# Attention levels 2+3 and 4+5 of a chunked linear attention as one TensorE pass each

## The reference, cut to what matters

```python
def _attn_ref(r, k, v, w, u):        # (2, 8, 768, 48) each, u (8, 48)
    ...
    for t in range(S):
        kt, vt, rt, wt = (k[:, :, t], v[:, :, t], r[:, :, t], w[:, :, t])
        cur = np.einsum('bhd,bhe->bhde', u[None] * kt, vt)
        y[:, :, t] = np.einsum('bhd,bhde->bhe', rt, state + cur)
        state = wt[:, :, :, None] * state + np.einsum('bhd,bhe->bhde', kt, vt)

def _moe_ref(x, w_in, w_out):        # (1536, 384) x (384, 2048) x (2048, 384)
    h = np.maximum(x @ w_in, 0.0)
    return (h * h) @ w_out

def _moe2_ref(x, w_gate, w1, w2, capacity):
    ...                              # argmax of 8 experts, at most 384 rows each
    h = np.maximum(np.einsum('ecd,edf->ecf', disp, w1), 0.0)
    y = np.einsum('ecf,efd->ecd', h, w2)
    ...                              # rows back to their places, times the gate's value
```

## Time and profile before

| | us |
|---|---|
| median of 3 runs | 453.12 (451.08 to 453.23) |
| the profiled execution, its own time | 450.08 |
| its span, first to last instruction | 448.1 |
| TensorE matmuls busy | 427.2 (95%) |
| VectorE busy | 303.9 (68%) |
| ScalarE busy | 257.7 (58%) |
| GpSimd busy | 57.0 (13%) |

### The profile page before, as it was taken

One profiled execution on the slowest core, in us unless ns is written; L12 is line 12 of the kernel. 1 busy time (PEld: TensorE's weight loads), 2 busy tenths in 40 slices (PEclk: granted clock), 3 DMA queues, 4 the chain that ended last, 5 costly groups with the idle time before them and its releaser, 6 DMA issues.

```text
span 448.1 us, 14525 instructions
## 1 busy us (share of the span) xinstructions
PE 427.2 (95%) x5882; PEld 405.4 (90%) x5882; DVE 303.9 (68%) x763; ACT 257.7 (58%) x527; POOL 57.0 (13%) x77
## 2 busy tenths in 40 slices
PE   2899999999999999999999999999999899999994
PEld 2778999999999999999999999989997789999994
DVE  4996966766777767777778637558538877687510
ACT  3366766546644664466546665573648875686421
POOL 6400000000000200010001000301030333421201
PEclk9999999999999999999999999999999999999998
DMA  6847976850400131010001094522885998520001
GB/s 217 287 145 241 354 260 237 312 222 3 170 29 1 39 132 66 1 39 2 3 3 38 4 327 169 194 72 77 302 262 169 346 336 292 168 63 2 30 2 45
DMA packets 35642, 63.39 MB, mean 141 GB/s; under 512 B 3980, under 2 KB 21950, under 8 KB 35568
## 3 DMA queue, kind: packets, MB, share of 16 engines
q1 hardware_dynamic: 33120, 57.87, 38.0%
q0 software_dynamic: 2304, 4.47, 2.7%
q10 hardware_dynamic: 144, 0.00, 0.0%
HBM read 50.77 MB, written 14.19 MB: 145 GB/s over the span
## 4 chain that ended last, share of the span: by engine, by line
PE 87%; DVE 3%; issue 3%; ACT 2%; DMA 1%; POOL 1%; POOLq 0%; SPq 0%; DVEq 0%; ACTq 0%
PE bank L721 22%; PE bank L707 22%; PE bank L934 6%; PE pair L628 6%; PE bank L887 5%; PE pair L592 3%; PE pair L887 3%; PE pair L902 3%; PE bank L941 3%; PE bank L902 3%; PE pair L647 2%; PE pair L682 1%; DMA stage<-in_moe_w_in 1%; ACT W L973 1%; PE pair L934 1%
## 5 line engine op out<-in xcount | busy, mean ns | idle before, releaser
L707 PE MATMUL bank<-XH,W 128*128 128x256 f32 x576 | 118.7, 284 | 0.7 <-ACT RB L1077 0.7
L721 PE MATMUL bank<-W,GH 128*128 128x384 f32 x372 | 98.3, 345 | 0.0
L707 PEld LDWEIGHTS bank<-XH,W 128*128 128x128 f32 x576 | 94.9, 188 | 1.7 <-issue 0.9
L707 PE MATMUL bank<-XL,W 128*128 128x256 f32 x288 | 80.6, 280 | 0.0
L1280 DVE TENSOR_TENSOR GL<-GG,GH 128x256 fp32r<-128x256 f32 x96 | 40.4, 421 | 35.0 <-ACT GH L973 31.9
L1077 ACT ACTIVATE RB<-bank 128x256 f32<-128x256 f32 x96 | 36.6, 381 | 47.1 <-PE bank L707 46.0
L721 PEld LDWEIGHTS bank<-W,GH 128*128 128x128 f32 x372 | 61.7, 188 | 1.2
L721 PE MATMUL bank<-W,GL 128*128 128x384 f32 x186 | 62.6, 336 | 0.0
L973 ACT ACTIVATE GH<-GG 128x256 fp32r<-128x256 f32 x96 | 40.2, 418 | 34.1 <-PE bank L721 32.3
L707 PEld LDWEIGHTS bank<-XL,W 128*128 128x128 f32 x288 | 54.3, 189 | 0.0
L1217 DVE TENSOR_TENSOR KS<-KS 128x512 f32<-128x512 f32 x72 | 49.8, 693 | 6.1 <-PE pair L628 5.8
(11 more groups left out here) (164 smaller groups left out, 711.5 us busy)
## 6 DMA issues: line engine op xcount, KB each, us to landing
raw<-in_moe_w SPq DMA_DIRECT2D x23, 768.0 KB, 7.6
stage<-in_moe_w SPq DMA_DIRECT2D x9, 768.0 KB, 7.8
KS<-in_krw SPq DMA_DIRECT2D x12, 512.0 KB, 5.9
slots<-X SPq DMA_DIRECT2D x8, 579.0 KB, 6.5
VV<-in_v SPq DMA_DIRECT2D x12, 288.0 KB, 6.2
KS<-in_krw SPq DMA_DIRECT2D x12, 256.0 KB, 6.1
stage<-in_moe_w_in SPq DMA_DIRECT2D x4, 768.0 KB, 6.6
stage<-in_moe_w_out SPq DMA_DIRECT2D x4, 768.0 KB, 6.7
```

Source lines behind the costliest of these rows:

```text
L707: last = nc.tensor.matmul(bank[4 + f % 2][:, 0:2 * P], win[wa][:, c, f * P:(f + 1) * P], xa[:, c, :], start=n == 0, stop=n == 3 * KM - 1)
L721: last = nc.tensor.matmul(bank[6 + m][:, 0:DM], ga[(NF * g + f) % G3][:, cols], wout[wa][:, f, :], start=f == 0 and n == 0, stop=f == NF - ...
```

## The change

For groups 1 to 5, `two_levels(i, t, l)` takes the place of two levels, for l = 1 and l = 3 (PAIRS). A block of 4L tokens has quarters 0 to 3. The keys, decayed as for level l, meet three read quarters in one matmul of 96 moving columns per head and chunk: quarters 1 to 3 as they are (48 columns) and a second set from MIX[t] (48 columns), in which GpSimd has decayed the reads ahead (`reads_ahead`, two multiplies: quarters 2 and 3 into two places, then quarter 3 once more). VectorE's `select_pair` takes from the result with three predicated copies that wait for one another (3, 2 and 1 quarters, 384, 256 and 128 elements), with new masks mask4. The updates and totals stay as they were, one for each level. `two_levels` stands in slots 2 and 6 (levels were due in 1, 3, 5, 7); the updates of levels 2 and 4 in slots 3 and 7. Group 0 keeps its levels. GpSimd's program gets `group_ahead(n)`: groups 1 and 2 at the start of iteration 1, group g + 3 ahead of group g's scatters; the wait for the zeroed buffers moves to the first scatter. PAGE_PAD, semaphore steps on TensorE's queue in iteration 6, goes from 160 to 176. `pr` now shares the memory of `sc`.

```diff
-    PAGE_PAD = 160
+    PAGE_PAD = 176
...
-    LATER = (-1, 1, 3, 5, 7, 9, 10, 11, 12, 13)
+    LATER = (-1, 2, 3, 6, 7, 9, 10, 11, 12, 13)
+    PAIRS = (1, 3)
...
-            step(nc.gpsimd.tensor_tensor(mask[:, :, :], mask2[:, :, 0:C // 2], mask2[:, :, C // 2:C], ALU.add))
+            step(nc.gpsimd.tensor_tensor(mask[:, :, :], mask2[:, 1:, 0:C // 2], mask2[:, 1:, C // 2:C], ALU.add))
+            step(nc.gpsimd.tensor_tensor(low, mask2[:, 0, 0:C // 2], mask2[:, 0, C // 2:C], ALU.add))
...
+            def reads_ahead(n, t, l):
+
+                L, w = 1 << l, PAIRS.index(l)
+                done = 4 * (n - 1) + 2 * w
+                got = MIX[t].rearrange("p (g b j) -> p g b j", b=4, j=L)
+                x = KRW[t][n % 2][:, 0:XW].rearrange("p (g b j) -> p g b j", b=4, j=L)
+                td = totals(n, t, l).rearrange("p (g b o) -> p g b o", b=4, o=1)
+                pool.wait_ge(att[t], NSTEP * n + l)
+                pool.wait_ge(upd[t], NL * n + l)
+                pool.wait_ge(tot[t], NL * n + l)
+                nc.gpsimd.tensor_tensor(got[:, :, 1:3, :], x[:, :, 2:4, :],
+                                        td[:, :, 1:3, :].to_broadcast([P, XW // (4 * L), 2, L]),
+                                        ALU.mult).then_inc(ahead[t], 1)
+                pool.wait_ge(ahead[t], done + 1)
+                nc.gpsimd.tensor_tensor(got[:, :, 3, :], got[:, :, 2, :],
+                                        td[:, :, 1, :].to_broadcast([P, XW // (4 * L), L]),
+                                        ALU.mult).then_inc(ahead[t], 1)
...
             def body(i, attn, mlp, gate):
+                if i == 1:
+                    for n in (1, 2):
+                        group_ahead(n)
                 if gate:
                     g = i - 2
+                    if g + 3 < NG:
+                        group_ahead(g + 3)
...
+            def two_levels(i, t, l):
+
+                L = 1 << l
+                pe.wait_ge(ahead[t], 4 * (i - 1) + 2 * PAIRS.index(l) + 2)
+                pe.wait_ge(sel[t], NMASK * i + l)
+                x = KRW[t][i % 2]
+                apart = (2 - i % 2) * WIDTH - XW
+                n = C if (i, l) == (1, PAIRS[0]) else C - L
+                for q in range(HP):
+                    for h in range(2):
+                        for a in range(2):
+                            rows, c = slice(DP * a, DP * a + D), q * P + h * C
+                            to = half(h, a).start
+                            first = x[rows, c + L:c + L + 1]
+                            reads = bass.AP(first.tensor, first.offset,
+                                            [first.ap[0], [apart, 2], [4 * L, C // (4 * L)], [1, 3 * L]])
+                            last = nc.tensor.matmul(pair[t][to:to + n, a, q * P:q * P + 3 * C // 2],
+                                                    x[rows, XW + c:XW + c + n], reads, start=q == 0, stop=q == HP - 1)
+                last.then_inc(att[t], 2)
...
-                    elif k < NL:
+                    elif k < NL and (n == 0 or k == NL - 1):
                         level(n, t, k)
+                    elif k in PAIRS:
+                        two_levels(n, t, k)
...
+            def select_pair(i, t, l):
...
+                dve.wait_ge(att[t], NSTEP * i + l + 2)
+                dve.wait_ge(sel[t], NMASK * i + l)
+                if i == 1:
+                    dve.wait_ge(masked, 1)
+                take(1, 4, 0, 0).then_inc(part_sel[t], 1)
+                dve.wait_ge(part_sel[t], done + 1)
+                take(2, 4, 1, 0).then_inc(part_sel[t], 1)
+                dve.wait_ge(part_sel[t], done + 2)
+                take(3, 4, 1, 2).then_inc(sel[t], 2)
...
-                    if k < NMASK:
+                    if n > 0 and k in PAIRS:
+                        select_pair(n, t, k)
+                    elif n == 0 and k < NMASK:
                         select(n, t, k)
```

More of the change, by code:

```diff
@@ L116, in rwkv_moe_kernel @@
         mask2 = IN[0][0][:, :, :].rearrange("p h n -> p (h n)")[:, 0:NMASK * C].rearrange("p (l n) -> p l n", l=NMASK)
-        mask = sb("mask", [P, NMASK, C // 2], on=p1)
+        mask = sb("mask", [P, NMASK - 1, C // 2], on=p1)
+        mask4 = sb("mask4", [P, 2, 3 * C // 4], on=p1)
         eye = sb("eye", [P, C], on=p1)
@@ L206, in unsplit @@
             return x.rearrange("p (a b) -> p a b", a=parts)
-        made = sem("made")
+        made, masked = sem("made"), sem("masked")
         cleared = sem("cleared")
@@ L222, in rwkv_moe_kernel @@
         tot = [sem(f"tot{n}") for n in range(2)]
+        ahead = [sem(f"ahead{n}") for n in range(2)]
+        part_sel = [sem(f"part_sel{n}") for n in range(2)]
         sel = [sem(f"sel{n}") for n in range(2)]
@@ L512, in _ @@
             step(nc.gpsimd.tensor_tensor(eye[:, :], ident[:, 0:C], ident[:, C:P], ALU.add))
[L513 removed]
+            step(nc.gpsimd.tensor_tensor(mask[:, :, :], mask2[:, 1:, 0:C // 2], mask2[:, 1:, C // 2:C], ALU.add))
+            step(nc.gpsimd.tensor_tensor(low, mask2[:, 0, 0:C // 2], mask2[:, 0, C // 2:C], ALU.add))
             pool.wait_ge(cst, n_cst[0])
             odd = right_half(eye[:, :], 0)[:, :, 0]
[L516 removed]
+            nc.gpsimd.tensor_tensor(odd, odd, low, ALU.add).then_inc(made, 1)
             def first_totals(t, l):
@@ L531, in _ @@
                     first_totals(t, l)
+            step(nc.gpsimd.memset(wide4[:, :, :], 1.0))
+            pool.wait_ge(cst, n_cst[0])
+            for n, l in enumerate(PAIRS):
+                L = 1 << l
+                m = wide4[:, n, :].rearrange("p (g b j) -> p g b j", b=3, j=L)
+                step(nc.gpsimd.affine_select(out=m, in_=m, compare_op=ALU.is_ge, fill=0.0, base=0,
+                                             pattern=[[-4 * L, C // (2 * L)], [-L, 3], [0, L]], channel_multiplier=1))
+            pool.wait_ge(cst, n_cst[0])
+            for n, l in enumerate(PAIRS):
+                L = 1 << l
+                m = wide4[:, n, :].rearrange("p (g b j) -> p g b j", b=3, j=L)
+                step(nc.gpsimd.affine_select(out=m, in_=m, compare_op=ALU.is_ge, fill=0.0, base=L - 1,
+                                             pattern=[[4 * L, C // (2 * L)], [L, 3], [0, L]], channel_multiplier=-1))
+            pool.wait_ge(cst, n_cst[0])
+            nc.gpsimd.tensor_tensor(mask4[:, :, :], wide4[:, :, 0:3 * C // 4], wide4[:, :, 3 * C // 4:3 * C // 2],
+                                    ALU.add).then_inc(masked, 1)
             step(nc.gpsimd.memset(earlier[:, 0, :], 0.0))
@@ L1245, in select, with take @@
                     got.rearrange("p x (g j) -> p x g j", j=L)).then_inc(sel[t], 1)
+            def select_pair(i, t, l):
+                L, w = 1 << l, PAIRS.index(l)
+                done = 4 * (i - 1) + 2 * w
+                got = pair[t][:, :, :].rearrange("p a (q c) -> p (a q) c", q=HP)
+                to = AD[t][:, :, :].rearrange("p x (g b j) -> p x g (b j)", b=4, j=L)
+                m = mask4[:, w, :].bitcast(U32).rearrange("p (x g j) -> p x g j", x=1, j=3 * L)
+                def take(first, last, v, k):
+                    n = (last - first) * L
+                    return nc.vector.copy_predicated(
+                        to[:, :, :, first * L:last * L], m[:, :, :, 0:n].to_broadcast([P, H, C // (4 * L), n]),
+                        got[:, :, 3 * C // 4 * v:3 * C // 4 * (v + 1)].rearrange(
+                            "p x (g j) -> p x g j", j=3 * L)[:, :, :, k * L:k * L + n])
+                dve.wait_ge(att[t], NSTEP * i + l + 2)
[7 more added lines that the diff above has]
+                take(3, 4, 1, 2).then_inc(sel[t], 2)
             def heads(x):
```

14 lines of the change are left out of this document (11 added, 3 removed).

## The result

The changed kernel takes **464.06 us** (median; 461.92 to 466.57, 4 runs) against 453.11 us for the kernel before: a ratio of 1.0264, with a 95% interval from 1.0227 to 1.0302. It is 2.6% slower. The prediction said 451.8 us, with a range of 448.0 to 455.0, and gave 0.11 to "slower".

A forecast was written before the change was run, and what follows sets the result against it. TensorE, 95% busy, was taken as the bound, unless VectorE came late. Against the profiled 450.08 us: + 0.2 + 1.2 - 1.5 - 3 x 0.4 = -1.3, so 448.8, on the median's footing 451.8 us; range 448.0 to 455.0.

The forecast's parts named there:

- Until kk_rows (slot 10) may read the second tile: Iterations 3 to 5: VectorE's gapless queue up to kk_rows takes 11.8 us, against TensorE's 10.7.
- A: Moment at which the first tile's pass for levels 4+5 (slot 6) is done; both engines' times count from it.
- The wait at kk_rows: Iterations 3 to 5: TensorE waits about 1.1 us for VectorE before the transposes of kk_rows; none in iteration 2.
- the -0.4 for each of iterations 3 to 5: Net gain per iteration: 1.52 us saved on TensorE less a wait of 1.1 at kk_rows.
- the saving: TensorE per group: two wide passes take 3.06 us where four levels took 4.58, so 1.52 less; all kept in iteration 2.
- GpSimd against VectorE: GpSimd's multiplies slow a VectorE update by at most 0.04 us, mostly in slack; taken as 0.
- lock: Rival, 9%: shared-port lock makes VectorE's queue in iteration 1 2 us later; +2.0, total 453.8 us.
- Iteration 1: VectorE's queue delays level 5 and project(6), which follows at 58.05 instead of 56.85: +1.2 us, give or take 0.5.
- The pass: TensorE's wide pass of 64 records with 96 moving columns: 21 ns a record (16.1 to 25.8), 1.34 us plus 0.19.
- The trio: VectorE's three new dependent selects: 1.25 us against 0.68 for two old ones, 0.1 more for levels 2+3.
- The prologue: Preamble: one more small GpSimd add ahead of `made`, on which the first select waits: +0.2 us (0.1 to 0.3).
- 96 columns bind TensorE: Rival, 8%: two quadrants at once make 37 ns a record, a pass 2.4 us plus 0.19; total 459 us.

The follow-up runs named there:

- e1: Changed kernel with choice, ranks and place of groups 0 to 2 moved from slots 7, 8, 9 to 12, 13, 14: 455.22 us, ratio 1.0074.
- e5: Changed kernel with the late place of e1, and GpSimd's scatter of groups 0 and 1 held until the next group's first passes are through: 453.32 us.
- e2: Changed kernel with 12 unread products put ahead of the first tile's level 5 in iterations 3 to 5: 463.48 us.
- e8: The kernel of e2 with TensorE's empty instructions of iteration 6 cut from 176 to 101: 458.56 us, ratio 1.0154.
- e4: Changed kernel without GpSimd's multiplies ahead of the passes (decays on 48 of 96 read columns left out): 462.07 us, ratio 1.0225.
- e7: Kernel before with only late choice, ranks and place, and the scatter of groups 0 and 1 behind the next first passes: 454.60 us, ratio 1.0040.

## Why the prediction was wrong, step by step

**The step that failed** is "Until kk_rows (slot 10) may read the second tile": it follows VectorE's queue to kk_rows and compares only there. TensorE has an earlier appointment with the same queue, level 5's wait for `place`. The prediction's own figures would have shown it. VectorE from A to the end of `place`: 2.29 + 1.95 + 0.48 + 1.2 + 1.74 + 1.30 + 1.08 = 10.04 us. TensorE from A to level 5: 147.38 - 137.32 = 10.06 before, less level 4 and a slot, plus half a pass: 10.06 - 1.03 - 2.11 + 0.47 = 7.39. Lateness 2.65 us; measured, 2.25. VectorE's share held: from the start of the trio to the end of `place` it took 10.23 us (143.18 to 153.41). Before, `place` was 0.3 us early. The wait was written out in the code, and in the trace of before it didn't show, because it was met.

**The wait at kk_rows**, forecast at 1.1 us, is zero in the changed kernel, which the prediction itself named as a sign of being wrong: the wait at level 5 had already made TensorE late. With `place` moved (e1, e5) it is zero too; 2.3 us had left the queue, more than the 1.1 (argued from the sum, not tested by itself). So the -0.4 for each of iterations 3 to 5 should have read 2.65 - 1.52 = +1.1, ahead of any clock; iteration 5, which lost no clock, came to +1.9. Most of the rest is the saving, which was smaller than 1.52: iteration 2, without a wait, gained 0.9, and -0.9 + 2.25 + 0.27 (a new wait ahead of the ranks, L843) = +1.6.

**The clock** had no place in the sum. In iterations 3 and 4 TensorE waited 2.25 us and then also got 1.2 GHz for some 3.4 us, 1.6 us lost each time (e2, e8). With it iterations 3 and 4 came to +3.5 and +3.3.

**GpSimd against VectorE** was set to 0 on one row, 0.72 against 0.68. That row was a weak witness: when the update began at 11.60, the GpSimd instruction then running had only 0.11 us to go.

```profile
11.31 0.40 POOL L526 TENSOR_TENSOR KS<-KS 128x128 f32<-128x128 f32 x1
```

With 0.67 to go, the updates show up to 0.54 more. For iterations 2 and 3 the zero holds on the span (e4), and for 4 and 5 once the clock is allowed for; for iteration 1 not: some 1.2 us by e8 against e4 at full clock, where the rival "lock" said 2.0 and had 9%. **Iteration 1** without the multiplies is 45.56 - 44.28 = +1.3, against +1.2 forecast; the remaining 1.4 of its 3.9 go with the stretch at 0.50, which the sum had no term for, and with what this iteration varies by. The hold behind the weight DMA and ScalarE, which the prediction read at 41.87, lasted until 43.61, in an iteration that began 1.4 us later. Its wait for GL ahead of project(2) was there, 1.77 for 1.7.

**The pass** takes 1.48 us (132.04 to 133.52, 142.23 to 143.70), 23.1 ns a record; I took 21, in a range of 16.1 to 25.8. The estimate from the Trainium skill's rule ("TensorEngine Tiling (Array Packing)", section Instruction Overhead) was 25.8; the measurement lies between. With 1.48 us a pass the sum puts iteration 2 at -1.25; it measured -0.9 against before and -1.2 against e7. **The trio** takes 1.37 us from its start to the update (143.18 to 144.55), 1.25 said, and for levels 2+3 it takes 1.79 (133.00 to 134.79), 1.35 said. **The prologue** lost 1.4 for +0.2; the step of which I spoke, the added instructions ahead of `made`, delays the first select by 0.6 (8.19 against 7.63), and the rest is within what that stretch varies by.

The rival "96 columns bind TensorE", the only one on the slower side, was not what happened: a pass took 1.48 us where it says 2.4. The right rival, *the queue makes `place` late*, wasn't among them.

## What to carry to other kernels

When an engine's queue gets longer, list every wait on it by the other engines in order, the satisfied ones too, and give each its margin; the first that turns negative sets the price, not the last or the most familiar. Buffers lent out for a side job (here the ranks in a tile's bank) are where such waits hide. And a wait of TensorE can cost more than its length, as it did here in seven of nine cases, so an optimisation that makes TensorE's work smaller and its partner's larger has to be placed, not only added up: the same wide passes are worth -0.4% or +2.6%, depending on where thirteen tiny instructions and a scatter stand, and on whether group 1 takes part.

## What the runs showed of the hardware

- With a stop of 2.24 or 2.25 us in the midst of work, TensorE's granted clock stood at 0.50 for some 3.4 us, or in two cases some 6.8, in seven of nine cases, beginning between 0.7 us before it resumed and 1.8 us after; filled with unread products, the clock stayed at 1.00 in six of six.
- 64 records of first-level products took 1.16 us alone and 3.12 and 2.94 us beside two indirect DMAs of GpSimd, in pieces; out of their way, 1.16 again. That they keep TensorE from its instructions is my reading; shown is only that the gaps come and go with them.
- 36 products more in TensorE's program brought 4.5 us of waits 200 us later, which went away when 75 empty instructions were taken out ahead of the place (the products are 72 instructions, with three waits).
- A multiply of 512 elements a partition on VectorE took 0.69 us alone and 1.23 where one of GpSimd had begun 0.09 us ahead of it; in the row of 0.72 the GpSimd instruction had 0.11 us to go.
